# Attention with the values held still and the heads in two column halves, in a three-stage kernel

## What is computed

```python
    scores = scale * np.matmul(q, k.transpose(0, 1, 3, 2))
    keep = is_sink | in_window            # first 4 keys, or 0 <= rel < 128
    scores = np.where(keep, scores, -1000000000.0)
    a = np.exp(scores - np.max(scores, axis=-1, keepdims=True))
    a = a / (np.sum(a, axis=-1, keepdims=True) + 1e-09)
    x = np.matmul(a, v)                   # heads side by side: (B, S, 512)
    theta = x @ w_theta
    u = x + einsum(w_tok_r, x*cos(theta)) + einsum(w_tok_i, x*sin(theta))
    m = u + np.maximum(u @ w_ch, 0.0)
    gate = sigmoid(causal convolution of m, 5 taps)
    out = (gate * (m @ w_val)) @ w_out
```

## Time and profile before

| what | value |
| --- | --- |
| median of 3 runs | 698.45 us (697.0 to 701.43) |
| the profiled execution | 698.34 us |
| its span | 696.5 us |
| granted PE clock, mean | 0.983 of full |
| busy: PE, PEld, DVE, ACT, POOL | 665.1, 590.4, 413.3, 290.7, 254.8 us |
| end of attention's loop work (last `normalise`) | 190.8 us |

### The profile page before, as it was taken

The page is one execution under the profiler, slowest core; times in us unless marked ns, Lnnn a source line. Parts: engine busy times, 40 slices in busy tenths (PEclk is TensorE's granted clock), DMA queues, the critical chain, the costliest instruction groups (busy, mean ns, idle before and its releaser), DMA issues.

```text
span 696.5 us, 14151 instructions
## 1 busy us (share of the span) xinstructions
PE 665.1 (95%) x4096; PEld 590.4 (85%) x4096; DVE 413.3 (59%) x992; ACT 290.7 (42%) x759; POOL 254.8 (37%) x327
## 2 busy tenths in 40 slices
PE   5999999999847999999999999999999999999996
PEld 4888888888735888888888888889989999999995
DVE  3667766767517444565456545786984575576460
ACT  4667667666414323232323232443432442343331
POOL 5535454454302212121212121225553454445321
PEclk9999999999969999999999999999999999999999
DMA  6455647465231122432233224623142201211111
GB/s 230 132 183 177 204 164 223 156 209 158 87 116 46 32 61 76 130 97 60 75 128 98 60 75 136 197 92 105 43 155 76 90 32 62 91 51 43 42 45 46
DMA packets 60021, 74.60 MB, mean 107 GB/s; under 512 B 4176, under 2 KB 41040, under 8 KB 59984
## 3 DMA queue, kind: packets, MB, share of 16 engines
q1 hardware_dynamic: 59984, 74.15, 33.2%
HBM read 48.97 MB, written 25.17 MB: 106 GB/s over the span
## 4 chain that ended last, share of the span: by engine, by line
PE 67%; issue 2%; DVE 1%; DMA 1%; ACT 1%; POOL 0%; POOLq 0%; SPq 0%; DVEq 0%; ACTq 0%
PE acc L1335 29%; PE ps_p L1384 17%; PE ps_o L1423 10%; PE ps_th L1324 10%; PE ps_x L1313 2%; DMA x_res<-xT_scratch 1%; POOL g_lo L1012 0%; DVE k_big L1167 0%; DVE xT_lo L1156 0%; DVE k_big L1162 0%; ACT xT_raw L1039 0%; POOLq L720 0%; ACT xT_hi L1041 0%; DVE k_int L1165 0%; DVE u_sb L1202 0%
## 5 line engine op out<-in xcount | busy, mean ns | idle before, releaser
L980 POOL TENSOR_TENSOR z_lo<-z_raw,z_hi 128x512 fp32r<-128x512 f32 x48 | 62.1, 1314 | 215.4 <-ACT z_hi L1054 215.4
L1335 PE MATMUL acc<-w2h,z_hi 128*128 128x512 f32 (+1 forms) x384 | 131.2, 342 | 0.0
L1335 PE MATMUL acc<-w2l,z_hi 128*128 128x512 f32 (+1 forms) x384 | 129.3, 337 | 0.0
L1335 PE MATMUL acc<-w2h,z_lo 128*128 128x512 f32 (+1 forms) x384 | 129.3, 337 | 0.0
L259 ACT ACTIVATE probs<-masked,neg_max 128x260 f32<-128x260 f32 (+1 forms) x192 | 92.6, 484 | 60.3 <-DVE neg_max L308 60.0
L308 DVE CUSTOM_DVE_ANT_0 masked<-ps_s,mask 128x260 f32<-128x260 f32 (+1 forms) x192 | 68.9, 402 | 53.0 <-PE ps_s L383 49.8
L1335 PEld LDWEIGHTS acc<-w2h,z_lo 128*128 128x128 f32 x384 | 72.8, 190 | 8.0
L1335 PEld LDWEIGHTS acc<-w2l,z_hi 128*128 128x128 f32 x384 | 72.9, 190 | 7.8
L1335 PEld LDWEIGHTS acc<-w2h,z_hi 128*128 128x128 f32 x384 | 72.8, 190 | 7.8
L1156 DVE TENSOR_TENSOR xT_lo<-ps_x,xT_hi 128x512 fp32r<-128x512 f32 x24 | 16.6, 691 | 95.6 <-ACT xT_hi L1041 95.5
L425 PE MATMUL ps_o<-v_sb,probsT 128*128 128x64 f32 x384 | 66.5, 268 | 0.0
(11 more groups left out here) (94 smaller groups left out, 1464.4 us busy)
## 6 DMA issues: line engine op xcount, KB each, us to landing
k_sb<-kT SPq DMA_DIRECT2D x16, 396.0 KB, 5.2
q_sb<-qT SPq DMA_DIRECT2D x16, 384.0 KB, 4.8
v_sb<-vP SPq DMA_DIRECT2D x16, 384.0 KB, 3.2
x_scratch<-x_sb SPq DMA_DIRECT2D x16, 384.0 KB, 4.2
x_nat<-x_scratch SPq DMA_DIRECT2D x24, 256.0 KB, 2.9
xT_scratch<-xT_raw SPq DMA_DIRECT2D x24, 256.0 KB, 2.2
x_res<-xT_scratch SPq DMA_DIRECT2D x24, 256.0 KB, 3.1
uT_scratch<-u_sb SPq DMA_DIRECT2D x24, 256.0 KB, 2.6
```

What stands on the lines that cost most here:

```text
L980: nc.gpsimd.tensor_tensor(z_lo[s % ZR][:, part, :], z_raw[:, part, :], z_hi[s % ZR][:, part, :].bitcast(F32), ALU.subtract).then_inc(z_lo_ ...
L1335: last = nc.tensor.matmul(bank, l, r, start=first and s == 0 and m == 0 and a == 0, stop=s == T - 1 and m == 1 and a == 2, skip_group_chec ...
```

## The change

The product with the values is turned round. The values (128 keys x 64 channels of a head) become the stationary operand and `probsT` is streamed, 256 or 128 columns at a time; head 0 writes partitions 0 to 63 and head 1 partitions 64 to 127 of one bank `ps_y`. So the output has channels on the partitions and queries along the free dimension. DVE (visits 0 and 2) and ACT (visit 1) copy `ps_y` to `y_sb`, and `turn_y` transposes it back into `ps_o`. There is one `sink_probs` and one `sinkT` for both heads, and one sink product for each tile from tile 2 on, added onto the transposed block. `vS` now fills all 128 partitions (256 KB a pair, twice as much), and the zeroing is gone. SP loads `q` and `k` of pair n+1 ahead of the other operands of pair n. `normalise` takes tiles 0 and 1 and then tiles 2 to 5, both heads in an instruction. Last, `outputs` waits for `g_lo` block by block.

```diff
-                for e in range(2):
-                    if m == 0:
-                        wait_count(pe, normed, 2 * (n - 1) + e + 1)
-                    pe.wait_ge((evac_v, evac_a)[e], k + 1)
-                    cols = slice(D * e, D * (e + 1))
-                    for i in (2 * m, 2 * m + 1):
-                        out = ps_o[e][:, i * D:(i + 1) * D]
-                        last = nc.tensor.matmul(out, probsT[e][:, i, P:2 * P], v_sb[s][:, i, cols],
-                                                start=i == 0, stop=i == 0, skip_group_check=True)
-                        if i >= 1:
-                            last = nc.tensor.matmul(out, probsT[e][:, i, 0:P], v_sb[s][:, i - 1, cols],
-                                                    start=False, stop=i == 1, skip_group_check=True)
-                    last.then_inc(pv_done, 1)
...
+                    wait_count(pe, y_evac[VISITS - 1], n)
+                else:
+                    pe.wait_ge(y_evac[m - 1], n + 1)
+                pe.wait_ge(evac_v, k + 1)
+                pe.wait_ge(evac_a, k + 1)
+                at = 2 * m * 2 * P
+                passes = [(2 * m, at + P, 0, 2 * P), (2 * m + 1, at + 3 * P, P, P)]
+                if m > 0:
+                    passes.append((2 * m - 1, at, 0, P))
+                for a, (j, src, dst, width) in enumerate(passes):
+                    for e in range(2):
+                        rows = slice(D * e, D * (e + 1))
+                        keysT = probsT[e][:].rearrange("p t k -> p (t k)")[:, src:src + width]
+                        last = nc.tensor.matmul(ps_y[rows, dst:dst + width], v_sb[s][:, j, rows], keysT,
+                                                start=a == 0, stop=a == len(passes) - 1, skip_group_check=True)
+                last.then_inc(pv_done, 1)
+
+            def turn_y(n, s, m):
+
+                if m < 2:
+                    wait_count(pe, normed, 2 * n + m)
+                pe.wait_ge(y_evac[m], n + 1)
+                if m > 0:
+                    pe.wait_ge(v_ready, n + 1)
+                    pe.wait_ge(sink_evac, n + 1)
+                for t in range(2):
+                    out = ps_o[:, (2 * max(m - 1, 0) + t) * P:(2 * max(m - 1, 0) + t + 1) * P]
+                    last = nc.tensor.transpose(out, y_sb[m][:, t * P:(t + 1) * P], ident[:])
+                    if m > 0:
+                        last = nc.tensor.matmul(out, sinkT[:], v_split[s][:, 2 * (m - 1) + t, :],
+                                                start=False, stop=True, skip_group_check=True)
+                last.then_inc(y_turned, 1)
...
                        qk(n, s, v, it + 1)
+                        if started:
+                            pv(n - 1, 1 - s, v, it + s)
                         if v > 0:
                             turn(n, v - 1, sinks=v == 1 and started)
                         elif started:
                             turn(n - 1, VISITS - 1, False)
-                        if v == 2:
-                            pv(n, s, 0, it + 1)
-                        elif started:
-                            pv(n - 1, 1 - s, v + 1, before)
+                        if v == 0 and not first:
+                            turn_y(n - 2, s, VISITS - 1)
+                        if v > 0 and started:
+                            turn_y(n - 1, 1 - s, v - 1)
...
-                pe.wait_ge(g_lo_done, CB * n + CB)
                 for j in range(UT):
                     wait_count(pe, o_evac, UT * n + max(j - 1, 0))
                     bank = ps_o[(UT * c + j) % 2]
                     for kk in range(CB):
+                        if j == 0:
+                            pe.wait_ge(g_lo_done, CB * n + kk + 1)
```

More of the change, by code:

```diff
@@ L109, in attention_fast @@
         ps_t = [ps(f"ps_t{e}", [P, 2, 2 * P]) for e in range(2)]
-        ps_o = [ps(f"ps_o{e}", [P, 512]) for e in range(2)]
+        ps_y = ps("ps_y", [P, 512])
+        ps_o = ps("ps_o", [P, 512])
         q_in = [early.q_in, sem("q_in1")]
@@ L128, in attention_fast @@
         v_ready = sem("v_ready")
-        sink_evac = [sem(f"sink_evac{e}") for e in range(2)]
+        sink_evac = sem("sink_evac")
         turned = sem("turned")
@@ L135, in attention_fast @@
         pv_done = sem("pv_done")
-        sunk = sem("sunk")
+        y_evac = [sem(f"y_evac{m}") for m in range(VISITS)]
+        y_turned = sem("y_turned")
         norm_step = sem("norm_step")
@@ L318, in evac, with evac_y @@
                                           ps_t[0][:].rearrange("p t k -> p (t k)")[:, P:4 * P]).then_inc(evac_v, 1)
[L320 to L324, removed]
+            def evac_y(n, m):
+                dve.wait_ge(pv_done, VISITS * n + m + 1)
+                wait_count(dve, y_turned, VISITS * (n - 1) + m + 1)
+                nc.vector.tensor_copy(y_sb[m][:], ps_y[:, 0:2 * P]).then_inc(y_evac[m], 1)
             def invert(n, s):
@@ L331, in invert, with normalise @@
                 nc.vector.reciprocal(inv_sum[:, s], row_sum_g[:, s]).then_inc(norm_step, 1)
-            def normalise(n, s, n_before):
-                for e in range(2):
[L335 to L341, removed]
+            def normalise(n, s, n_before, first_tiles):
+                tiles = slice(0, 2) if first_tiles else slice(2, T)
+                count = tiles.stop - tiles.start
+                dve.wait_ge(y_turned, VISITS * n + (1 if first_tiles else VISITS))
+                dve.wait_ge(norm_step, 2 * n + 2)
+                wait_count(dve, x_out[s], 16 * n_before)
+                inv = inv_sum[:, s].rearrange("p e t -> p t e")[:, tiles].unsqueeze(3)
+                nc.vector.tensor_tensor(x_sb[s][:, tiles, :].rearrange("p t (e d) -> p t e d", d=D),
+                                        ps_o[:, 0:count * P].rearrange("p (t e d) -> p t e d", e=2, d=D),
+                                        inv.to_broadcast([P, count, 2, D]), ALU.mult).then_inc(normed, 1)
             def step(it, first=False):
@@ L345, in step @@
                     n = 2 * it + s
+                    started = not (first and s == 0)
                     for v in range(VISITS):
                         k = VISITS * n + v
-                        if v == 2 and not (first and s == 0):
-                            normalise(n - 1, 1 - s, it if s == 1 else it - 1)
                         for t in range(2):
@@ L352, in step @@
                                 mask_max(n, s, v, t, e)
-                        if v == 1 and not (first and s == 0):
-                            evac_sinks(n - 1)
-                        if not (first and s == 0 and v == 0):
+                        if v == 1 and not first:
+                            normalise(n - 2, s, it - 1, False)
+                        if v == 2 and started:
+                            normalise(n - 1, 1 - s, it if s == 1 else it - 1, True)
+                        if v != 1 and started:
+                            evac_y(n - 1, v)
+                        if started or v > 0:
                             evac(k - 1, (v - 1) % VISITS)
-                        if v == 1 and not (first and s == 0):
+                        if v == 1 and started:
                             invert(n - 1, 1 - s)
@@ L399, in turn @@
                     free_turn_bank(e, k)
[L400 to L403, removed]
+                    if e == 1 and m == 1:
+                        wait_count(pe, sink_evac, n)
+                    if e == 1 and sinks:
+                        turn_sink(n - 1)
                     for t in range(2):
```

105 lines of the change are left out of this document (54 added, 51 removed).

## The result

The changed kernel takes 676.92 us (median of 4, 675.52 to 677.93), the kernel before 697.73 beside it: a ratio of 0.9699, 95% interval 0.9645 to 0.9753. The forecast was 678, from 669 to 703.

What follows compares the result with a forecast made beforehand. PE was taken to bound the attention pairs. Pairs -12.4, start -4.9, end of attention +1 and last outputs -3.8 sum to -20.1 us on 698.34: 678 us, range 669 to 703.

Steps and rivals of the forecast that it cites:

- The bound: Attention pairs: PE was taken to be busy throughout, 11.13 us a pair, against 7.87 for DVE and 7.52 for ACT.
- The turned product: Products with the values: fp32 at half speed, column halves side by side, 2.35 us a pair plus 0.45 for entering the mode.
- Rival 2: Values in attention: the column halves run in a row, PE's sum 12.0 to 12.3 us a pair, 707 us; chance 0.16.
- rival 3: Attention pairs: halves side by side but weight loads exposed, 11.4 us a pair, 695 us; chance 0.08.
- PE's sum: Attention pair: PE's work without waits sums to 9.65 us, against 11.13 before.
- The 0.34 for every third passage: Third passage of each visit: 0.34 us in place of 0.15, a pair 0.6 us longer, the kernel at 686 us.
- DVE's waits: Visits 1 and 2 of a pair: DVE's order makes PE wait, 0.65 us a pair, giving 10.3 us.
- Rival 1: Attention pairs: halves side by side but hand-overs bind, 0.4 us a visit, 10.9 a pair, 687 us; chance 0.16.
- The start: Before pair 1: loading its k earlier removes the 2.94 us pause and the long records behind it, -4.9 us.
- Rival 4: Start and outputs: pause isn't the load, or PE's clock drops; each other case moves +2 to +7 us; no separate chance.
- The end of attention: From the last scores to the last normalise's end: a longer chain, about 11 us for 9.97, +1 us.
- the outputs: Last unit: nine of 36 products fill the gap before the outputs and long records go, -3.8 us.

## Why the prediction was right

**The bound.** Right: PE bound the pair before and binds it after; doubled transposes reach the end in full.

**The turned product.** Right, to 0.03 us: 2.83 a pair for 2.35 + 0.45. Both assumptions under it held, the half speed of fp32 and the overlap. They are shown by the run with head 0 twice. The reading that led to them was weaker than the result. The 132 ns between a record of 260 fp32 columns and one of 256 rounded ones would by themselves give 1.0 ns a column and not 0.83. And the count of records in flight depends on where in the product one looks: in the `qk` at 102.96 it is two for the first 0.3 us and four only in later pieces, one of which the forecast took. In the run with heads in a row, what differs at the start is the count, two side by side and one in a row. Rival 2 (in a row, 707 us) and rival 3 (bare loads, 695) are out. Of the statements of the Trainium skill, TensorE: Matmul & The Clock Gate, Part 3, the one on several column tiles at once agrees with these runs. The one that a weight load overlaps only with products in another row group does not. All products of L450 share the 128 rows, and six bare loads at the forecast's 0.11 us would add 0.66 to the 0.85 of visit 1's values, which take 1.02 in all.

**PE's sum.** 9.65 was forecast without waits. The pair of 10.04 less its wait of 0.22 is 9.82, so the sum was 0.17 short, in the passages and visit 0's scores (0.97 in every second pair, 0.86 in the others); the run without the wait has 9.87. The 0.34 for every third passage, by which the kernel would have been at 686, is not borne out: one passage more cost 0.13 in visit 2 and 0.05 to 0.16 in visit 0.

**DVE's waits.** This is the mis-sized term: 0.65 a pair in the forecast, 0.22 in the trace. DVE's own busy time was put too high as well, 8.4 a pair for a measured 8.06. The place was right (`turn_y` in visit 1 behind the larger `normalise`), and moving `normalise` takes it away; but in visit 2 it does not occur, and nothing followed from it. With the 0.17 this made the pairs 10.04 and not 10.3, 14 pairs 14.6 us shorter and not 11.6. Rival 1 (10.9 a pair) put it higher still.

**The start.** The pause was the load, as argued, and the scores of visit 1 came even earlier than forecast (14.85, not 16). But the sum ended there. The forecast looked at POOL's slack in the steady part (5.6 us a pair) and left out that at the start POOL is late. Its split of the sinks waits for their load until 11.02, then come two weight splits of 3.1 us together, and only then the gather, which ends at 17.66. In the kernel before it ended at 16.35, and nobody waited for it, as pair 1's scores began only at 15.88. Visit 1 took 6.42 and not 3.3. To visit 2 of pair 1 the gain was 3.8 and not 5.7. Rival 4 had said that this end could fail; it named other mechanisms.

**The end of attention, the outputs.** +0.7 for +1, and -3.6 for -3.8.

**Together** the miss at the start, +1.9, and +0.6 in tokens and channels, which no edit aims at, stood against -3.0 in the pairs. The total, -20.7 in the span for -20.1, is nearer than its terms are: that it came within 0.6 is luck. That it came out faster, and near 3%, is not; the turned product, the outputs and the load of `k` carry it.

## What to carry to other kernels

When the operand with 64 columns is made the stationary one, count what each product streams and in which column half it lies: here two halves side by side cost the time of the fuller one, as long as the program changes halves after at most four records. An engine that is busy to 100% still has its own time to give back; in this kernel the sum of its parts was a good forecast (9.65 for 9.82), better than the guess about hand-overs (0.65 for 0.22). A wait taken away at the start can uncover the next one: follow the sum until both kernels are in their steady part.

## What the runs showed of the hardware that was not expected

PE starts a product in the other column half ahead of program order over a short distance: with four records of one half ahead of it nothing was lost (0.81 us in visit 0 of the run with heads in a row, 1.02 in visit 1 of the next), with six visit 1's values took 1.51. What lies at five, and whether loads count, wasn't tried.

PE's wait for `probs` of pair 1 was followed by a lower clock in some traces and not in others. After 1.8 us (changed kernel), 2.4 (transposes first), 1.9 (heads four records apart) and 1.3 (`normalise` first) it was granted mostly 1.2 GHz for 3.3 to 6.6 us. After 1.05 (`y_sb` twice), 0.8 (heads in a row) and 0.3 us (head 0 twice), and in the two runs without the wait, the same stretch stood at 2.4 GHz throughout.
